# A one-core chain of attention and two mixtures of experts: x turned at another place in memory, w1's split in sixteen pieces, idle products in four waits

## The reference

```python
# 1. attention: batch 2, 8 heads, 576 positions, head size 64
cum = np.cumsum(np.maximum(s, 0.0), axis=-1)
scores = np.where(causal, -1e9, scale * q @ k.T + np.minimum(-(cum_i - cum_j), 0.0))
attn = exp(scores - max); attn /= attn.sum(-1) + 1e-9;  x = attn @ v      # x: 1152 tokens x 512
# 2. mixture of 8 experts, the best two of each token (512 -> 1024 -> 512)
noisy = x @ w_gate + np.log1p(np.exp(x @ w_noise)) * noise
top2 = the two largest of noisy; weights = softmax over the two
for e: out[mask] += weight * (np.maximum(x[mask] @ w1[e], 0.0) @ w2[e])
# 3. 8 dense experts, their shares balanced in 8 rounds (rows, then columns)
P = exp(logits - max); 8 times: P /= P.sum(1); P /= P.sum(0); P *= N / E
for e: out += P[:, e:e+1] * (np.maximum(x @ w1[e], 0.0) @ w2[e])
```

## Time and profile before

| what | us |
|---|---|
| median of 3 runs | 1260.33 |
| the three runs | 1258.71, 1260.33, 1322.38 |
| the profiled execution | 1261.05 |
| its span, first to last instruction | 1259.3 |
| PE busy in the span | 1216.9 |
| DVE, ACT, POOL busy | 486.3, 365.0, 153.7 |
| mean granted TensorE clock | 0.982 |

### The profile page before, as it was taken

How to read it: one execution, slowest core, us unless ns; L and a number is a source line. 1 busy time by engine, 2 the same in 40 slices (tenths; PEclk the granted TensorE clock), 3 DMA queues, 4 the chain that set the end, 5 groups by cost and what they waited for, 6 DMA issues and landing times.

```text
span 1259.3 us, 17471 instructions
## 1 busy us (share of the span) xinstructions
PE 1216.9 (97%) x6611; PEld 1082.8 (86%) x6611; DVE 486.3 (39%) x1089; ACT 365.0 (29%) x702; POOL 153.7 (12%) x227
## 2 busy tenths in 40 slices
PE   8999399999999699999999999999999999999998
PEld 5888288888888589999999999999999999999997
DVE  6554475554544432442133133233234214214321
ACT  5665244444444241131122122122122113112110
POOL 8767011111102530000000000000000000000000
PEclk9999699999999899999999999999999999999999
DMA  7760634444446530011011011012002101100000
GB/s 173 170 167 11 235 112 176 164 161 152 168 173 206 183 142 1 1 68 67 1 67 67 0 67 67 0 41 93 0 0 73 60 0 67 67 0 0 25 25 25
DMA packets 23968, 102.98 MB, mean 82 GB/s; under 512 B 4590, under 2 KB 9198, under 8 KB 19962
## 3 DMA queue, kind: packets, MB, share of 16 engines
q1 hardware_dynamic: 17498, 85.97, 20.5%
q0 software_dynamic: 3360, 11.01, 3.0%
q10 hardware_dynamic: 3072, 5.51, 1.3%
HBM read 87.74 MB, written 10.30 MB: 78 GB/s over the span
## 4 chain that ended last, share of the span: by engine, by line
PE 92%; POOL 2%; DVE 2%; DMA 1%; ACT 1%; issue 1%; POOLq 0%; DVEq 0%
PE bank L734 14%; PE bank L733 14%; PE bank L732 14%; PE bank L714 14%; PE bank L715 14%; PE bank L716 14%; PE bank L664 3%; PE bank L613 1%; PE bank L647 1%; PE bank L648 1%; PE bank L766 1%; POOL w1l L518 1%; DMA x_sb<-x_dram,gather_at 1%; POOL q_two L502 0%; PE bank L678 0%
## 5 line engine op out<-in xcount | busy, mean ns | idle before, releaser
L714 PE MATMUL bank<-xTh,w1h 128*128 128x384 f32 (+1 forms) x1024 | 344.1, 336 | 3.0 <-DVE xTl L1173 1.6
L715 PE MATMUL bank<-xTl,w1h 128*128 128x384 f32 (+1 forms) x1024 | 342.1, 334 | 0.0
L716 PE MATMUL bank<-xTh,w1l 128*128 128x384 f32 (+1 forms) x1024 | 341.5, 333 | 0.0
L977 ACT ACTIVATE hh<-bank 128x384 fp32r<-128x384 f32 (+1 forms) x256 | 123.5, 482 | 657.7 <-PE bank L716 657.7
L734 PE MATMUL bank<-w2h,hl 128*128 128x512 f32 (+1 forms) x768 | 303.1, 395 | 0.0
L733 PE MATMUL bank<-w2l,hh 128*128 128x512 f32 (+1 forms) x768 | 301.2, 392 | 0.0
L732 PE MATMUL bank<-w2h,hh 128*128 128x512 f32 (+1 forms) x768 | 300.5, 391 | 0.0
L1193 DVE SCALAR_TENSOR_TENSOR hl<-bank,hh 128x384 fp32r<-128x384 f32 (+1 forms) x256 | 139.5, 545 | 371.1 <-ACT hh L977 371.0
L714 PEld LDWEIGHTS bank<-xTh,w1h 128*128 128x128 f32 x1024 | 193.6, 189 | 5.5 <-issue 2.0
L715 PEld LDWEIGHTS bank<-xTl,w1h 128*128 128x128 f32 x1024 | 193.7, 189 | 1.2
L716 PEld LDWEIGHTS bank<-xTh,w1l 128*128 128x128 f32 x1024 | 193.6, 189 | 0.0
(11 more groups left out here) (171 smaller groups left out, 679.2 us busy)
## 6 DMA issues: line engine op xcount, KB each, us to landing
raw<-in_w SPq DMA_DIRECT2D x15, 2048.0 KB, 8.0
raw<-in_w1b SPq DMA_DIRECT2D x8, 2048.0 KB, 7.7
raw<-in_w2b SPq DMA_DIRECT2D x8, 2048.0 KB, 7.7
k_raw<-in_kT SPq DMA_DIRECT2D x16, 288.0 KB, 5.3
y_dram<-x_sb ACTq DMA_DIRECT2D x16, 256.0 KB, 3.5
q_raw<-in_qT SPq DMA_DIRECT2D x8, 288.0 KB, 5.0
q_two<-w2l SPq DMA_DIRECT2D x8, 288.0 KB, 6.0
x_dram<-x_sb SPq DMA_DIRECT2D x1, 2304.0 KB, 9.2
```

The source lines that it names most:

```text
L714: pe.matmul(dst, w1h[:, c, fs], xTh[:, c, ts], start=(c == 0), stop=False)
L715: pe.matmul(dst, w1h[:, c, fs], xTl[:, c, ts], start=False, stop=False)
L716: mm = pe.matmul(dst, w1l[:, c, fs], xTh[:, c, ts], start=False, stop=(c == DC - 1))
L977: act.activation(hh[:, f, 0:n_cols], bank[:, f % UP_BANKS, 0:n_cols], ACT.Relu).then_inc(st.hh_ready, 1)
```

## The change

Three edits. (1) The order in which attention's buffers are given out is changed, and `xTh` and `xTl` come directly behind `raw2`, 16,384 bytes into the region: over `k_raw`, `q_raw`, the running sums and `q_two`. `hh`, `hl` and `x2` move up by the same 36,864 bytes. No instruction is added or moved by this; the first turned tile stays at step 76 (`ALL - ST`). (2) ACT's eight roundings of w1 come one a step in steps 61 to 68, and POOL's subtraction is cut into sixteen pieces of 256 columns in steps 64 to 79. (3) `stay_warm(n, bank)` issues n fp32 products of `ones` (128x128) with `ident` (128 columns) into a bank that is free there: 18 behind the gate's logits, 20 behind the ranks, 18 behind the lists of expert 0, 29 ahead of the three turned tiles of the dense stage. Nobody reads them.

```diff
+        q_two = sb("q_two", [P, Q_RING, N], F32R, where=attn)
+        unused = sb("unused", [P, 2, S], F32R, where=attn)
+        causal = sb("causal", [P, BANK + P], where=attn)
+        probT = sb("probT", [P, UNIT_RING, PROBS], where=attn)
...
         raw2 = sb("raw2", [P, FC, DM])
+        xTh = sb("xTh", [P, DC, N], F32R)
+        xTl = sb("xTl", [P, DC, N], F32R)
         hh = sb("hh", [P, FC, BLK], F32R)
...
+        WARM_TOP2, WARM_RANKS, WARM_GATHER, WARM_BACK = 18, 20, 18, 29
-        W1_LOW_AT, EARLY_AT, GATES_AT = 71, 76, 60
+        W1_LOW_AT, EARLY_AT, GATES_AT = ALL - 4 * DC, ALL - ST, 60
...
-            return (h, *divmod(part, 2)) if h > 1 and part < 4 else None
+            if h == H and part < 2 * DC:
+                return (h, *divmod(part, 2))
+            return (h, *divmod(part, 2)) if 1 < h < H and part < 4 else None
...
-            def low_w1(c, half):
-                cols = slice(half * F // 2, (half + 1) * F // 2)
-                pool.wait_ge(SP_.w1h_ready, c + 1)
-                part = pool.tensor_tensor(w1l[:, c, cols], raw1[:, c, cols], w1h[:, c, cols].bitcast(F32), ALU.subtract)
-                if half:
-                    part.then_inc(SP_.w1_ready, 1)
+            def low_w1(c, part):
+                cols = slice(part * F // LOW_CHUNKS, (part + 1) * F // LOW_CHUNKS)
+                if part == 0:
+                    pool.wait_ge(SP_.w1h_ready, c + 1)
+                done = pool.tensor_tensor(w1l[:, c, cols], raw1[:, c, cols], w1h[:, c, cols].bitcast(F32), ALU.subtract)
+                if part == LOW_CHUNKS - 1:
+                    done.then_inc(SP_.w1_ready, 1)
...
-                if k >= W1_LOW_AT and k - W1_LOW_AT < 2 * DC:
-                    low_w1((k - W1_LOW_AT) // 2, (k - W1_LOW_AT) % 2)
+                if k >= W1_LOW_AT:
+                    low_w1(*divmod(k - W1_LOW_AT, LOW_CHUNKS))
...
+            def stay_warm(n, free_bank):
+                for _ in range(n):
+                    pe.matmul(bank[:, free_bank, 0:P], ones[:], ident[:], start=True, stop=True)
...
+            stay_warm(WARM_TOP2, Y0)
             pe.wait_ge(ranks_in, 1)
...
+            stay_warm(WARM_RANKS, Y0)
             lists(0)
+            stay_warm(WARM_GATHER, Y0)
             turn_gathered(0, False)
...
+            stay_warm(WARM_BACK, UP_BANKS - 1)
             for t in range(BLK_T):
                 pe.wait_ge(x2_ready, t + 1)
                 turn_token(DN, t, x2)
...
-                    if h >= H:
-                        high_w1(2 * (h - H) + of, half)
+                    if h == H:
+                        high_w1(of, half)
```

More of the change, by code:

```diff
@@ L110, in build @@
         k_two = [w2h_flat[:, i * N:(i + 1) * N] for i in range(HEADS_RING)]
[L111 to L118, removed]
         k_raw = sb("k_raw", [P, RAW_RING, N], where=attn)
@@ L125, in build @@
         cum_l = sb("cum_l", [P, S], F32R, where=attn)
+        q_two = sb("q_two", [P, Q_RING, N], F32R, where=attn)
+        unused = sb("unused", [P, 2, S], F32R, where=attn)
+        causal = sb("causal", [P, BANK + P], where=attn)
+        probT = sb("probT", [P, UNIT_RING, PROBS], where=attn)
+        v_sb = sb("v_sb", [P, V_RING, STEPS, VW], where=attn)
+        aug = sb("aug", [P, MAX_RING, STEPS, 2], F32R, where=attn)
+        rinv = sb("rinv", [P, 2, STEPS], where=attn)
+        ident_r = sb("ident_r", [P, P], F32R, where=attn)
         attn.close()
         raw2 = sb("raw2", [P, FC, DM])
+        xTh = sb("xTh", [P, DC, N], F32R)
+        xTl = sb("xTl", [P, DC, N], F32R)
         hh = sb("hh", [P, FC, BLK], F32R)
@@ L141, in build @@
         colE = [sb(f"colE{i}", [P, E]) for i in range(2)]
-        xTh = sb("xTh", [P, DC, N], F32R)
-        xTl = sb("xTl", [P, DC, N], F32R)
         gate_rows = [x2[:].rearrange("p t d -> p (t d)")[0:4 * E, 0:N],
```

## The result

| what | before | after |
|---|---|---|
| median, us | 1260.33 | 1253.67 (1251.67 to 1254.22, 5 runs) |
| ratio after / before | | 0.9954, 95% interval 0.9938 to 0.9970 |
| profiled execution | 1261.05 | 1254.22 |
| its span | 1259.3 | 1252.5 |
| mean granted clock | 0.982 | 0.994 |

By the ratio the change saves 0.46%, 5.8 us (0.0046 x 1260). Some executions of most kernels here take 1271 to 1322 us (the three of them with a trace show TensorE's clock at half for tens of microseconds in attention); the comparisons by medians leave out all above 1265 us and call the others undisturbed, and the last experiment is about the long ones.

The account below looks back on a forecast made before the run. The chain of waits is 92% PE, with waits ended by DVE and gathers. From the profiled 1261.05: -0.43 - 0.1 - 0.5 - 0.5 - 0.8 = -2.3, giving 1258.7 us; range 1254.5 to 1263.

Parts of the forecast that it names:

- The place in memory: Moving `xTh` and `xTl` adds no instruction, wait or transfer and starts none earlier: costed at nothing.
- the surprise: A changed pace of the products that read `xTh` and `xTl`, 0.15 us apart at full clock; no chance given.
- The split of w1: Last steps of attention: earlier roundings and POOL pieces of 0.73 us remove PE's waits of 0.27 and 0.16 us, -0.43 us.
- The price of an idle product: In the four waits: 0.22 us each at full clock, 0.43 at half, all ending inside their waits, cost 0.
- (a): The ranks, ten small products from 141.36 us, run at full clock: -0.1 us.
- (b): Ahead of expert 0, the third turned tile, the only one on the chain, is turned at full clock: -0.5 us.
- (c): The third turned tile of the dense stage is turned at full clock: -0.5 us.
- (d): First sparse and dense `up` products: half pace costs 1.9 and 2.1 us; none expected back, taken as 0.
- The rival in which the clock holds: Idle products and tiles keep full clock up to both first `up`s: -4.0 us more, sum 1254.7 us; chance 12%.
- (e): Clock dip at 480 us, which lost 1.6 us, may be absent in another execution: half taken, -0.8 us.
- Products that become the wait: Clock stays at half during the idle products, so 18, 20 and 18 overrun their waits: 1268.4 us; chance 8%.
- POOL's pieces setting the pace: End of attention: pieces of 0.9 us or more make cuts lag PE, the -0.43 is gone: 1259.1 us and up; chance 4%.

Follow-up runs that it names:

- the last experiment: Changed kernel with 64 bytes ahead of `xTh` and idle products between turned tiles, plus three idle products ahead of `mix(0)`: median 1253.83 us, ratio 0.9947.
- 128, 128: Changed kernel with 64 unused bytes ahead of `xTh`, so `xTh` and `hh` both at remainder 128 by 256 bytes: 1248.06 and 1251.04 us, two others 1278.59 and 1283.18.
- 128, 0: Changed kernel with 64 unused bytes ahead of `xTh` and 128 more ahead of `hh` (remainders 128 and 0 by 256 bytes): 1295.85 us, clock at half for 81.9 us.
- 0, 64: The kernel before, unedited, `xTh` at remainder 0 by 256 bytes and `hh` at 64: median 1260.33 us.

## Why the prediction was right and wrong

The time, 1253.67, lies below the range of 1254.5 to 1263.0 by 0.8 us (the ratio would put it at 1254.5); in the ratio, 5.8 us of gain against a forecast of 1.6 to 2.3. "Within 2%" was right. That it came out so close to the range is luck: the lower end stood for a clock that holds through both first `up`s, which did not happen, and the largest term was taken as nothing.

- **The place in memory: the step that failed.** "I cost it at nothing." It is -5.5 us in the dense stage and +1.3 in the sparse one, between the two profiled executions. The kernel with the places alone is 4.9 us faster than before, by the medians of undisturbed runs. The step asked only which instruction would start earlier. The page of the profile counts 3 x 1024 `up` and 3 x 768 `down` products, so that 3 ns a product are 7 to 9 us. A changed pace was named as "the surprise" and given no chance. It should have been a rival with both signs. By the table, over some 22 dense stages, the pairs tried lie between -7.6 us (128, 128: 22 x -0.22 and 23 x -0.12) and +0.9 (128, 0: 22 x -0.22 and 23 x +0.25), against 0, 64.
- **The split of w1: mechanism right, size off.** Both waits went, nothing took their place, the piece was 0.726 us for the 0.73 estimated. The term was -0.43 and measured -1.04. The wait shown before an instruction is no measure of what it costs: the starts of the turned tiles moved by 0.61 us more than the two marks together. From the first turned tile to the second it was 1.65 us (118.40 to 120.05) and is 1.11, with a mark of 0.27 for these 0.54 us; from the second to the third it was 1.71 and is 1.28, with a mark of 0.16 for these 0.43.
- **The price of an idle product**: 0.235 to 0.24 us, forecast 0.22, and no wait was overrun.
- **(a)** -0.12 for -0.1, right. **(b)** -0.46 for -0.5, right, and the tiles were turned at full clock: the rule of the Trainium skill (TensorE: Matmul & The Clock Gate, Part 4: PE-mode transpose), by which turns don't count as work in the way products do, did not bring the clock down before the third tile here. It was down 1.9 us behind it, at 156.3. **(c)** about -0.3 for -0.5 (from DVE's third `x` to the first `up`, 3.01 us for 3.32).
- **(d)** taken as 0, and 0 it is: both first `up`s still start at half clock, 20.60 us for 20.50 and 26.25 for 26.29. The rival in which the clock holds didn't happen. With the gaps between the tiles filled it did at both, in one profiled execution; at the dense `up` it did in two executions without that, too. The advice of the same page of the Trainium skill (Why this matters for your kernels), to leave no idle gaps between bursts, agrees with the traces at the first sparse `up` (five falls in five with open gaps, none in two with filled ones); at the dense one they don't decide. The 1.9 us that the prediction put on the first sparse `up` were too much, since a later gather takes back three quarters or all of it; of the 2.1 us on the dense one 1.4 came in.
- **(e)** The fall at 480 was forecast half; it was gone, -1.57, and one at 176.8 us came, +1.37. Net -0.2 for -0.8. Neither is shown to be the change's doing: of the 14 traces nine have the fall some 40 us behind the first dense `up` and five don't, with the new places alone among the five; and five have the other, the old order with 128 bytes ahead of `xTh`, which has no added product, among them.

Products that become the wait, and POOL's pieces setting the pace, didn't happen: the nearest wait had 0.57 us left. The price of the first of these rivals was too low in the prediction: at 0.43 us the 29 products ahead of the dense stage would take 12.5 us against a wait of 7.52, another 5 us that its 1268.4 leaves out.

## What to carry to other kernels

Where products of one kind fill the time, compare their start-to-start distances between two builds before anything else; a buffer that moves by 64 bytes can outweigh what the edit was made for, with either sign, and a pad is a cheap thing to sweep once all else is fixed. Cost a wait on TensorE by the starts of the work behind it, not by the idle time shown. An idle product pays only where it keeps the clock into a burst of real work that no other wait stops: at the first sparse `up` the clock held once the short gaps were filled too, and it gained half a microsecond at most; at the first dense one it was worth 1.4 us, but held in some executions without that. So judge such an edit over many executions.

## What the runs showed of the hardware

- An fp32r product of 384 columns stands 175.9 ns from the next, on average, with `xTh` at a remainder of 0 by 256 bytes (and `hh` at 64), 173.3 ns at 64; 96 of them take 16.64 to 16.96 us by the two addresses. The `down` products, 72 in a stage, take 16.32 to 16.73.
- TensorE's clock fell from 2.4 to 1.2 GHz 1.2 to 2.4 us behind a stand of under 1 us and stayed there for 37 to 130 us of gapless work in attention, in three executions with a trace; 35 of 94 executions took over 1265 us, as these did, and none of twelve with three idle products in that stand.
- Where it was at half at the start of a first `up`, it came back 2.9 (no idle products) to 6.0 us behind the first of the large products.
- Two executions of one kernel without any long fall differ by up to 5.8 us (1258.17 to 1263.94 over the eight with the old places; 1253.14 to 1258.0 over the last experiment's twelve).
